# Two transitions of a fused attention and feed-forward kernel: another order on VectorE, ScalarE and GpSimd

## The reference

```python
mask = q_bucket[:, :, :, None] == k_bucket[:, :, None, :]
scores = np.where(mask, scale * np.matmul(q, k.transpose(0, 1, 3, 2)), -1e9)
attn = softmax(scores)                      # 16 heads of 768 x 64
x = (attn @ v) laid out as 1536 x 512
h = x @ w_in                                # 512 x 2048
x = (h - np.tanh(h)) @ w_out                # 2048 x 512
for e in range(4):                          # 512 x 1024 and 1024 x 512 each
    h = np.maximum(x @ w1[e], 0.0)
    out += p[:, e:e + 1] * (h @ w2[e])
```

## Time and profile before

| | |
|---|---|
| median of 3 runs | 1011.68 us (1010.9 to 1012.18) |
| profiled execution | 1011.95 us, its span 1010.2 us |
| TensorE busy | 988.7 us, 98% |
| VectorE, ScalarE, GpSimd busy | 67%, 46%, 44% |
| attention | to about 244 us |
| first layer | 244 to about 513 us, first passage 244 to 282 us |
| experts | to the end, second passage 484 to 540 us |

### The profile page before, as it was taken

One profiled execution on the slowest core, in us unless ns is written; L12 is line 12 of the kernel. 1 busy time (PEld: TensorE's weight loads), 2 busy tenths in 40 slices (PEclk: granted clock), 3 DMA queues, 4 the chain that ended last, 5 costly groups with the idle time before them and its releaser, 6 DMA issues.

```text
span 1010.2 us, 16473 instructions
## 1 busy us (share of the span) xinstructions
PE 988.7 (98%) x5408; PEld 910.3 (90%) x5408; DVE 672.5 (67%) x1119; ACT 463.1 (46%) x850; POOL 443.4 (44%) x434
## 2 busy tenths in 40 slices
PE   6999999999999999999999999999999999999998
PEld 4889898988899999999888989889899898998987
DVE  5888888887865546555887555655556555556555
ACT  4887888887544344343543313223142232322321
POOL 3677779997575373553634304113041230412200
PEclk9999999999999999999999999999999999999999
DMA  5566566563102002010010100101001010010002
GB/s 133 151 167 167 159 181 165 158 171 89 32 16 59 22 21 62 10 52 21 21 57 19 52 22 21 63 21 42 21 21 62 21 42 21 21 63 21 21 18 106
DMA packets 50724, 65.40 MB, mean 65 GB/s; under 512 B 5408, under 2 KB 32128, under 8 KB 50688
## 3 DMA queue, kind: packets, MB, share of 16 engines
q1 hardware_dynamic: 50528, 64.58, 22.4%
q10 hardware_dynamic: 160, 0.39, 0.1%
HBM read 44.07 MB, written 3.19 MB: 47 GB/s over the span
## 4 chain that ended last, share of the span: by engine, by line
PE 87%; DVE 6%; issue 3%; ACT 2%; POOL 1%; DMA 1%; SPq 0%; ACTq 0%; DVEq 0%; POOLq 0%
PE ps L1493 32%; PE ps L1516 25%; PE ps L1524 11%; PE ps L1440 6%; PE ps L1410 6%; PE ps L1421 5%; PE ps L1384 2%; DVE xq_lo L1073 1%; DVE pT_lo L1029 1%; DVE xq_raw L1061 1%; DVE hb L1190 0%; ACT pT_hi L735 0%; DMA k_raw<-in_kT 0%; DMA proj_raw<-in_proj 0%; DVE prob L1022 0%
## 5 line engine op out<-in xcount | busy, mean ns | idle before, releaser
L1493 PE MATMUL ps<-xq_hi,wu_lo 128*128 128x384 f32 x672 | 227.0, 338 | 2.0 <-DVE xq_lo L1073 1.1
L1493 PE MATMUL ps<-xq_hi,wu_hi 128*128 128x384 f32 x672 | 226.2, 337 | 0.0
L1493 PE MATMUL ps<-xq_lo,wu_hi 128*128 128x384 f32 x672 | 226.0, 336 | 0.0
L1221 DVE SCALAR_TENSOR_TENSOR acc<-ps,p_norm,acc 128x512 f32<-128x512 f32 x180 | 134.9, 749 | 101.3 <-PE ps L1516 95.8
L584 POOL TENSOR_TENSOR wu_lo<-wu_raw,wu_hi 128x768 fp32r<-128x768 f32 (+1 forms) x48 | 103.8, 2184 | 222.0 <-ACT wu_hi L771 222.0
L1516 PE MATMUL ps<-wd_lo,g_hi 128*128 128x512 f32 x384 | 150.9, 393 | 0.0
L1516 PE MATMUL ps<-wd_hi,g_hi 128*128 128x512 f32 x384 | 150.9, 393 | 0.0
L1516 PE MATMUL ps<-wd_hi,g_lo 128*128 128x512 f32 x384 | 150.6, 392 | 0.0
L1493 PEld LDWEIGHTS ps<-xq_hi,wu_lo 128*128 128x128 f32 x672 | 126.1, 188 | 8.0 <-ACT hb L842 1.7
L1493 PEld LDWEIGHTS ps<-xq_lo,wu_hi 128*128 128x128 f32 x672 | 126.2, 188 | 3.9
L919 ACT ACTIVATE g_hi<-hb 128x384 fp32r<-128x384 f32 x96 | 50.4, 525 | 165.6 <-DVE hb L1179 100.7
(11 more groups left out here) (121 smaller groups left out, 1756.0 us busy)
## 6 DMA issues: line engine op xcount, KB each, us to landing
wu_raw<-in_w SPq DMA_DIRECT2D x64, 128.0 KB, 3.0
wd_raw<-in_w SPq DMA_DIRECT2D x16, 512.0 KB, 3.4
q_raw<-in_qT SPq DMA_DIRECT2D x32, 192.0 KB, 3.3
k_raw<-in_kT SPq DMA_DIRECT2D x30, 192.0 KB, 3.3
wu_raw<-in_w_in SPq DMA_DIRECT2D x32, 128.0 KB, 2.3
wd_raw<-in_w_out SPq DMA_DIRECT2D x8, 512.0 KB, 3.5
v_raw<-in_vP SPq DMA_DIRECT2D x16, 192.0 KB, 2.8
inv_rows<-inv_dram SPq DMA_DIRECT2D x16, 192.0 KB, 3.2
```

The source lines that it names most:

```text
L1221: dve.scalar_tensor_tensor(out=part_of, in0=source, scalar=scale, in1=part_of, op0=ALU.mult, op1=ALU.add).then_inc(down_taken, 1)
L1493: mm = pe.matmul(to, w[:, wslot, k, :], x[:, xslot, k, :], start=start and k + m == 0, stop=k == 1 and m == 2, skip_group_check=not start)
```

## The change

The change moves instructions inside the two passages and moves one from VectorE to GpSimd. The work of all engines is the same but for that one, which becomes two.

- VectorE, block (0,0): `take_inverse` goes in front of `first`, and the second `last_sum` behind `hidden_sub` of part 1. On ScalarE the second `move_last` goes behind the tanh of part 1.
- The remainder `wd_lo` of group 1 is made by GpSimd as two operations of 128x512 (`down_rest` in the gpsimd block), in block (0,1) behind `x_rest` of slot 2.
- VectorE, block (0,1): `x_rest` of slot 3 goes in front of the move of down tile 5.
- VectorE, block (3,3): down tiles 3 and 4 and `hidden_sub` of part 1 go in front of `x_sum` of slot 4; `x_rest` of slot 1 and `hidden_sub` of part 2 go ahead of `x_rest` of slot 3, and that one ahead of down tile 5.
- VectorE, block (4,0): `x_rest` of slot 2 goes in front of `first`, down tile 0 in front of `x_sum` of slot 5, down tiles 3 and 4 in front of `x_rest` of slot 6.
- ScalarE: `take_c5` moves ahead in blocks (0,1), (0,2) and (4,2), behind `take_c1`.
- GpSimd: the four sums of the next group at the end of block (3,3) go behind the hidden remainder of part 3.

```diff
+                def down_rest(group, par):
+                    pool.wait_ge(wd_hi_ready, group + 1)
+                    for f in range(FC):
+                        rest = pool.tensor_tensor(wd[par][1][:, f, :], wd_raw[:, f, :],
+                                                  wd[par][0][:, f, :].bitcast(F32), ALU.subtract)
+                    rest.then_inc(wd_lo_ready, 1)
...
+                    if early is not None:
+                        down_rest(1, 1)
                     hidden_rest(i, r, 1, 0, 1, 1)
...
-                    stage1(I1 - 1, r)
+                    stage1(I1 - 1, r, sums=r < 3)
                 hidden_rest(I1 - 1, 3, 3, 1, 0, 3)
+                up_sums(2 * (I1 - 1) + 3)
...
                     take_c1(i, r, False)
+                    if ahead:
+                        take_c5(i, r, False)
...
-                    first()
                     if start:
                         take_inverse(HEADS - 1, 1, slots[1])
+                    first()
...
-                    if b is not None:
+                    if b == 1:
                         x_sum(b, 4)
                     if start:
                         third()
+                    if b == 2:
+                        down(3, 4)
+                    hidden_sub(i, r, 1)
+                    if b == 2:
+                        x_sum(b, 4)
+                    else:
+                        down(3, 4)
+                    if start:
                         last_sum(1)
-                    hidden_sub(i, r, 1)
-                    down(3, 4)
-                    if not start:
+                    else:
                         third()
                     if b == 2:
                         x_rest(b, 1)
-                    down(5)
+                        hidden_sub(i, r, 2)
                     if b is not None:
                         x_rest(b, 3)
-                    hidden_sub(i, r, 2)
+                    down(5)
+                    if b != 2:
+                        hidden_sub(i, r, 2)
...
+                    if c is not None:
+                        x_rest(c, 2)
                     first()
+                    down(0)
                     if c is not None:
                         x_sum(c, 5)
-                    down(0)
-                    if c is not None:
-                        x_rest(c, 2)
...
                     if c is not None:
+                        down(3, 4)
                         x_rest(c, 6)
                     positive_rest(i, r, 1, 0, 1)
```

More of the change, by code:

```diff
@@ L651, in hidden_rest, with stage1 @@
                                        ALU.subtract).then_inc(g_lo1_ready, 1)
-                def stage1(i, r, early=None, late=None):
+                def down_rest(group, par):
[4 more added lines that the diff above has]
+                    rest.then_inc(wd_lo_ready, 1)
+                def stage1(i, r, early=None, late=None, sums=True):
                     if not (isinstance(i, int) and i + r == 0):
@@ L677, in stage1 @@
                     hidden_rest(i, r, 2, 1, 1, 2)
-                    if r in (2, 3):
+                    if r in (2, 3) and sums:
                         up_sums(2 * i + r)
@@ L857, in free_hidden, with stage1 @@
                     act.wait_ge(down_full, first_tile(pi, pr, psecond))
-                def stage1(i, r, a=None, b=None, late=None):
+                def stage1(i, r, a=None, b=None, late=None, ahead=False):
                     start = isinstance(i, int) and i + r == 0
@@ L878, in stage1 @@
                     take_tanh(i, r, 0, hb[:, 0, :])
-                    take_c5(i, r, False)
+                    if not ahead:
+                        take_c5(i, r, False)
                     if not (isinstance(i, int) and i == 0 and r < 2):
@@ L896, in stage1 @@
                     take_c2(i, r, False)
-                    if start:
-                        move_last(1)
                     act.wait_ge(h12_ready, count_of(i, r) + 1)
@@ L901, in stage1 @@
                     if start:
+                        move_last(1)
                         act.wait_ge(h22_ready, 1)
@@ L919, in positive, with stage2 @@
                     act.activation(to, u_ps[r % 2] if n == 3 else source, ACT.Relu).then_inc(g_hi_ready, 1)
-                def stage2(i, r, more=True, begins=False, a=None, b=None, c=None, late=None):
+                def stage2(i, r, more=True, begins=False, a=None, b=None, c=None, late=None, ahead=False):
                     pi, pr, _ = earlier(i, r, True, 1)
@@ L940, in stage2 @@
                         x_round(late, 5)
+                    if ahead:
+                        take_c5(i, r, True)
                     free_hidden(i, r, True)
@@ L944, in stage2 @@
                         x_round(c, 5)
-                    if not begins:
+                    if not begins and not ahead:
                         take_c5(i, r, True)
@@ L965, in _ @@
                 stage1(0, 0, a=1)
-                stage1(0, 1, b=1)
-                stage1(0, 2, late=1)
+                stage1(0, 1, b=1, ahead=True)
+                stage1(0, 2, late=1, ahead=True)
                 stage1(0, 3)
@@ L976, in _ @@
                 stage2(I1, 1, a=3, b=3)
-                stage2(I1, 2, late=3)
+                stage2(I1, 2, late=3, ahead=True)
                 stage2(I1, 3)
@@ L1272, in stage1 @@
                         down_rest(2 * i, 0)
-                    if r == 1:
+                    if r == 1 and b is None:
                         down_rest(2 * i + 1, 1)
@@ L1322, in stage2 @@
                     if c is not None:
+                        down(3, 4)
                         x_rest(c, 6)
                     positive_rest(i, r, 1, 0, 1)
-                    down(*((3, 4) if after1 else (3,)))
+                    if c is None:
+                        down(3)
                     third()
```

## The result

The changed kernel takes 1014.54 us, the median of ten runs (1013.11 to 1015.97). The kernel before, run beside it, takes 1011.67 (ten runs, 1010.9 to 1012.61). The ratio is 1.0026, interval 1.0016 to 1.0035. The forecast was 1013.1 in a range of 1008.0 to 1014.8, so the time lies in the range, but the kernel is slower by 2.9 us and not by the 1.4 forecast. The profiled execution of after took 1013.32 us, span 1011.5, against 1011.95 of before: 1.37 more.

A forecast was written before the change was run, and what follows sets the result against it. TensorE, busy 98% of the span, was taken as the bound. First passage -0.3, second +0.7 and clock +1.0 make +1.4 on 1011.68, so 1013.1 us, range 1008.0 to 1014.8.

The forecast's parts named there:

- The bound: TensorE bounds the kernel, full from 540 to 1000 us; only the two passages can pay, some 8 us at most.
- The rule of turns: VectorE and GpSimd alternate on two-SBUF-operand work; held VectorE operations end 0.41 (128x384) or 0.81 (128x768) after GpSimd.
- Rival 2: Block (4,0): GpSimd keeps its turn through four sums, ending at 503.4; clock holds, 1010.7 us; chance 0.13.
- First passage: Blocks (0,0) to (0,2): old stops go, new waits for tile 3 and GpSimd's hidden part come; net -0.3 us.
- the term of block (0,0): Block (0,0)'s edits and the early fifth-product copy bring down tile 2 of block (0,1) 0.5 us earlier.
- Second passage: Three stops go, but late sums delay c2 in block (4,0), 4.1 us idle; net +0.7 us without the clock.
- The clock: Block (4,0): after 4.1 us idle, 8 matmuls run at half speed, 1.4 us, 0.4 of it covered; +1.0.
- The sum: -0.3 for the first passage, +0.7 for the second and +1.0 for the clock, over both passages.
- rival 4: Same wait at slot 5, clock low through block (4,0), at least 12 matmuls at half speed; up to 1015.9; chance 0.13.

The follow-up runs named there:

- e5: Changed kernel with 24 unread matmuls of 384 columns in front of TensorE's wait for c2 in block (4,0): 1012.50 us, ratio 1.0006.
- e6: Changed kernel, sums still late, with ScalarE copying c2 ahead of both weight roundings in block (4,0): 1013.76 us, ratio 1.0026.
- e7: Changed kernel with GpSimd's four sums back in their old place and c2 copied ahead of both weight roundings in block (4,0): 1011.41 us, ratio 0.9998.
- e3: Changed kernel with 12 unread matmuls of 384 columns in front of TensorE's wait for c2 in block (4,0): 1013.13 us, ratio 1.0015.
- e8: e7 with the second last_sum back in front of hidden_sub of part 1 in block (0,0): 1010.60 us.
- e11: e6 with VectorE's third addition of block (4,0) moved directly behind down tiles 3 and 4: 1011.50 us, ratio 0.9998.
- e2: Kernel before with only GpSimd's four sums moved behind the hidden remainder of part 3: 1014.69 us, ratio 1.0029.
- e10: e7 with the third addition directly behind down tiles 3 and 4, e8's edit, and group 1's wd_lo back on VectorE: 1007.35 us, ratio 0.9962.

## Why the prediction was right, and where its size was off

**The bound.** Right: the blocks from 540 us on took 460.00 of 460.00 us, and both passages hold the whole difference.

**The rule of turns.** Right to 0.1 us. In after GpSimd's `wu_lo` ended at 253.17 and VectorE's subtraction beside it 0.42 later, in the timelines of the two:

```profile
250.77 2.40 POOL L584 TENSOR_TENSOR wu_lo<-wu_raw,wu_hi 128x1024 fp32r<-128x1024 f32 x1
...
251.99 1.60 DVE L1205 TENSOR_TENSOR hb<-hb,tanh_h 128x384 f32<-128x384 f32 x1
253.62 0.56 DVE L1152 TENSOR_TENSOR x_f<-ps,pv_other 64x384 f32<-64x384 f32 x1
```

The four sums too: alone 0.74, they took 1.57, 1.05 and 1.44 where VectorE got its turn between them, and 0.72 where it did not. Rival 2, that GpSimd keeps its turn, falls with these rows. The Trainium skill ("SBUF — State Buffer", "Who interferes with whom") calls this an exclusive lock that holds the loser for the whole instruction; these rows agree, and in them the engine that waited goes next, ahead of the other's following instruction.

**First passage, forecast -0.3, measured 0.0.** The mechanism was right: a stop of 1.06 for tile 3 stands where before had none (forecast, counted start to start, 1.17; measured 1.22), GpSimd's part came at 274.63 + 1.09 + 0.52 = 276.24 (forecast 275.92), and the 1.28 for `wd_lo` went. The halves of that remainder, for which no row stood in before, were to take 1.29 each. The first, held behind VectorE's sum to 267.37, could go on from 267.23. Since the subtraction behind it ended at 268.93, 0.41 after it, it ended at 268.52: 1.29. The timelines of GpSimd and VectorE:

```profile
266.50 3.57 POOL L657 TENSOR_TENSOR wd_lo<-wd_raw,wd_hi 128x512 fp32r<-128x512 f32 x2
...
265.70 1.67 DVE L1076 TENSOR_TENSOR xq_raw<-acc,xq_raw 128x768 f32<-128x768 f32 x1
267.29 1.64 DVE L1205 TENSOR_TENSOR hb<-hb,tanh_h 128x384 f32<-128x384 f32 x1
```

The start at 275.86 is thus the one forecast for `g_lo`, though the profile names another (see the result). The 0.3 was lost earlier, in the term of block (0,0): down tile 2 of block (0,1) came 0.21 earlier, not 0.50. The last sum ended 0.12 later than worked out, and I had not seen the 0.19 lost at 259.78 to c1, in front of the removed wait for c5.

**Second passage, forecast +0.7 without the clock.** The steps up to the last product of (4,0) held. The three stops at 492.16, 502.26 and 510.69 are gone. The sums ended at 504.62 + 0.50 = 505.12 (forecast 505.0), c2 was ready at 507.74 + 0.50 = 508.24 (508.15), the stop was 4.21 (4.1), and TensorE was 507.79 + 0.50 - 506.51 = 1.78 late at that product (1.74). The third addition ended at 512.42 + 0.50 = 512.92 (512.85). In e5, where the clock stays, the last product came 1.19 late (1.1) but (4,2) gave only 0.24 back (0.37), and the passage is 0.95 longer than before's, not 0.7.

**The clock, forecast +1.0.** In the profiled execution right: ten matmuls 0.32 apart and not eight, 10 x 0.15 = 1.5 us (forecast 1.4). The last product of (4,0) came 2.27 late (1.1 + 1.0 = 2.1 forecast) and (4,2) gave 0.41 back (0.37). Of the 1.86 us by which the passage is longer, 0.95 is the order, as e5 has it, and 0.9 the clock. In the median the term was half of what it is: e5 prices it at 2.0.

**The sum.** Against a forecast of 0.4 + 1.0 = 1.4, e5 splits the measured 2.9 into 0.9 for the order (1012.50 against the 1011.60 of before beside it) and 2.0 for the clock. So both terms were too small, the clock's most. Why other executions lose more than the profiled one was not seen, since only that one has a trace. After's ten runs spread over 2.9 us, e5's eleven over 1.3, which points to the clock term as what varies, but does not show it. The mean granted clock of whole executions does not settle it either: the three fastest of after's ten have 0.997 or 0.998, the others 0.994 to 0.996, but such a mean also takes in falls in the first 20 us that cost nothing visible (see the last section).

By its time the result is rival 4's: over 1013.70, and outside the forecast's own 1012.3 to 1014.2. It lies 0.26 under the upper end of the range. Whether the cause is rival 4's too, at least 12 matmuls at half speed, is shown for no execution; the profiled one had ten. That the time fell inside the range is in part luck: the size of the clock term was chosen between 0 and 4.2, and the reason given for a small one, that 2.14 us at the start had left the clock alone, does not bear it, as the last section shows.

**What the prediction did not ask.** It followed the chain from the sums to c2 and stopped, since that was what TensorE would wait for. e6 and e7 show that this names the stop, but not what removing it is worth: behind it stood the chain through x slot 6.

## What to carry to other kernels

When a wait is to be cut, list everything on each in-order queue between the late event and every consumer, not just the first consumer: here moving c2 alone gained nothing that can be told from noise (e6 and after both have a ratio of 1.0026), and c2 with one addition of 0.54 us took 3.0 us off the changed kernel (1011.50 for 1014.54). Work for the next group (sums, weight roundings) belongs behind what the present block waits for, but ahead of any wait in the same queue that is longer than the work itself: here four sums of 0.74 stood behind a wait of 3.72. A stop of two microseconds amid dense matmuls should be priced with the matmuls after it too: here 0.9 us in the profiled execution, 2.0 in the median.

## What the runs showed of the hardware that was not expected

TensorE's granted clock can fall after a short stop in one execution and not in another. After stops of 2.12 us (e3), 2.31 (e8), 4.21 (after) and 4.50 (e6), and after the two of 1.50 and 0.85 in e11, matmuls of 384 columns stood 0.32 us apart, the 1.2 GHz level, about ten of them; after 2.39 (e2) and the same 2.31 (e7) they did not. In after, e3, e6 and e8 the clock was still full when the stop ended and fell 0.3 to 1.4 us later, while TensorE was working again. The length of the stop alone does not decide it in these runs, and what does was not settled.

The start of the kernel shows the same. The stop of 2.14 us from the earlier trace rows stands in all thirteen traces, in code that no edit touches. In eight of them the clock was full up to 20 us; in five (e3, e5, e6, e8, e10) it was at half level for some of the time between 11 and 19 us. So that one row of before was one outcome of two, and not a length that the clock bears. Two windows, of before and of e5:

```profile
10.00:20.00 10.00, 6.28 (x36) 4.83 (x35) 6.41 (x11) 5.70 (x11) 4.63 (x4) 1.00 0.53 133
```

```profile
10.00:20.00 10.00, 7.86 (x37) 6.62 (x36) 5.66 (x10) 5.11 (x9) 5.07 (x6) 0.66 0.54 146
```

There the low clock costs nothing that can be seen: e5's first up product is at 243.04, before's at 243.86. The Trainium skill ("TensorE: Matmul & The Clock Gate", "Why this matters for your kernels") asks for no long idle between bursts. The runs agree as to the fall, and show that in some executions a stop of 2.12 us is long enough for it.
